# Attention by pair of heads and 192 tokens with stacked 64-query tiles; first layers in tiles of 192 and 384 tokens, second layers in 464; weights split in the first tile

## The reference

```python
def _attn_ref(q, k, v):                      # B, H, S, D = 4, 8, 576, 64; factor = 4
    q_d, k_d, v_d = (mean of each 4 tokens)  # 144 tokens
    out_up = np.repeat(sm_attn(q_d, k_d, v_d), factor, axis=2)
    mask = np.abs(pos[:, None] - pos[None, :]) < factor
    scores = np.where(mask, scale * np.matmul(q, k.transpose(0, 1, 3, 2)), -1e9)
    attn = softmax(scores)                   # divided by (sum + 1e-09)
    return out_up + np.matmul(attn, v)

def _moe_ref(x, w_in, w_out):                # 512 -> 2048 -> 512, ELU
    h = x @ w_in
    return np.where(h > 0, h, np.exp(np.minimum(h, 0)) - 1) @ w_out

def _moe2_ref(x, w_gate, w_val, w_out):      # 512 -> 1536 -> 512, SwiGLU
    g = x @ w_gate
    return (g / (1 + np.exp(-g)) * (x @ w_val)) @ w_out
```

## Time and profile before

| | |
|---|---|
| median of three runs | 1067.14 us |
| span of the profiled execution | 1064.6 us, clock 0.992 on average |
| the profiled execution's own time beside its span | not given apart; the median stands 2.5 us above the span |
| TensorE busy | 1020.6 us, 96% |
| DVE, ACT, POOL busy | 492.5, 383.6, 179.7 us |
| matmuls of first layers, 288 columns | 3072 |
| matmuls of second layers, 384 columns | 2592 |

### The profile page before, as it was taken

The page is one execution under the profiler, slowest core; times in us unless marked ns, Lnnn a source line. Parts: engine busy times, 40 slices in busy tenths (PEclk is TensorE's granted clock), DMA queues, the critical chain, the costliest instruction groups (busy, mean ns, idle before and its releaser), DMA issues.

```text
span 1064.6 us, 20019 instructions
## 1 busy us (share of the span) xinstructions
PE 1020.6 (96%) x7136; PEld 990.1 (93%) x7136; DVE 492.5 (46%) x1459; ACT 383.6 (36%) x1204; POOL 179.7 (17%) x207
## 2 busy tenths in 40 slices
PE   5499999899999999999999999999999999999998
PEld 4389999799998899999999999999999999999998
DVE  7856576365674555755644333223223232232222
ACT  5645344254453444545435622212212221221212
POOL 4740331001331012410007720000000000000000
PEclk9999999899999899999999999999999999999999
DMA  7621021111211111211034611000000001000000
GB/s 234 205 70 42 29 90 38 47 47 30 65 60 29 50 47 53 68 29 47 10 96 139 174 57 31 30 1 30 32 1 30 30 1 31 30 1 1 31 1 31
DMA packets 35146, 54.96 MB, mean 52 GB/s; under 512 B 3488, under 2 KB 23136, under 8 KB 35040
## 3 DMA queue, kind: packets, MB, share of 16 engines
q1 hardware_dynamic: 35040, 53.55, 16.7%
HBM read 44.10 MB, written 9.44 MB: 50 GB/s over the span
## 4 chain that ended last, share of the span: by engine, by line
PE 85%; DVE 6%; ACT 3%; issue 3%; DMA 1%; POOL 0%; SPq 0%; DVEq 0%; ACTq 0%
PE bank L314 26%; PE bank L315 25%; PE bank L316 25%; PE bank L274 3%; PE bank L300 2%; PE bank L285 1%; DVE g_sb L558 1%; PE bank L279 1%; PE bank L306 1%; ACT weights L704 1%; DVE prob L524 1%; DVE neg_max L509 1%; DVE v_pool L433 1%; DVE g_sb L560 1%; DVE prob L505 1%
## 5 line engine op out<-in xcount | busy, mean ns | idle before, releaser
L314 PE MATMUL bank<-x_hl,weights 128*128 128x384 f32 (+1 forms) x1088 | 352.1, 324 | 10.1 <-issue 9.6
L315 PE MATMUL bank<-x_hl,weights 128*128 128x384 f32 (+1 forms) x1088 | 347.5, 319 | 0.0
L316 PE MATMUL bank<-x_hl,weights 128*128 128x384 f32 (+1 forms) x1088 | 347.4, 319 | 0.0
L314 PEld LDWEIGHTS bank<-x_hl,weights 128*128 128x128 f32 x1088 | 206.2, 190 | 9.9 <-issue 8.7
L315 PEld LDWEIGHTS bank<-x_hl,weights 128*128 128x128 f32 x1088 | 206.5, 190 | 6.1 <-issue 6.1
L316 PEld LDWEIGHTS bank<-x_hl,weights 128*128 128x128 f32 x1088 | 206.3, 190 | 0.0
L314 PE MATMUL bank<-g_hl,weights 128*128 128x288 f32 x512 | 158.3, 309 | 1.5 <-DVE g_hl L566 1.5
L315 PE MATMUL bank<-g_hl,weights 128*128 128x288 f32 x512 | 152.7, 298 | 0.0
L316 PE MATMUL bank<-g_hl,weights 128*128 128x288 f32 x512 | 152.4, 298 | 0.0
L594 DVE TENSOR_TENSOR u_sb<-bank,u_sb 128x384 f32<-128x384 f32 x72 | 40.1, 557 | 199.3 <-ACT u_sb L744 199.3
L566 DVE TENSOR_TENSOR g_hl<-g_sb,g_hl 128x288 fp32r<-128x288 f32 x128 | 71.9, 562 | 86.6 <-ACT g_hl L681 86.6
(11 more groups left out here) (71 smaller groups left out, 1281.6 us busy)
## 6 DMA issues: line engine op xcount, KB each, us to landing
late_stages<-w SPq DMA_DIRECT2D x31, 256.0 KB, 3.2
v_win<-v_windows SPq DMA_DIRECT2D x32, 153.0 KB
q_sb<-qT SPq DMA_DIRECT2D x32, 144.0 KB, 2.2
k_sb<-kT SPq DMA_DIRECT2D x16, 288.0 KB, 3.0
v_raw<-v_rows SPq DMA_DIRECT2D x16, 288.0 KB
yT_scratch<-y_sb SPq DMA_DIRECT2D x32, 144.0 KB, 1.9
y_raw<-yT_scratch SPq DMA_DIRECT2D x6, 768.0 KB, 4.5
outT<-out_sb SPq DMA_DIRECT2D x24, 192.0 KB, 1.9
```

Source lines behind the costliest of these rows:

```text
L314: nc.tensor.matmul(bank[:, 0:n_cols], w_hi, x_hi, start=first, stop=False)
L315: nc.tensor.matmul(bank[:, 0:n_cols], w_hi, x_lo, start=False, stop=False)
L316: return nc.tensor.matmul(bank[:, 0:n_cols], w_lo, x_hi, start=False, stop=last)
```

## The change

Attention works on a unit: a pair of heads and 192 tokens, 48 units in all. The two heads of a pair are stacked on the 128 partitions, with 64 queries each, in three tiles with windows of 70 keys. One unit has 16 score instructions, 5 transposes of 128 columns and 20 output instructions. The mask is a tensor that DVE adds to the scores of all three tiles at once.

The prologue has only the first 4 units, the first 192 tokens. The first layers then run in seven tiles: 192, 192, and five of 384 tokens, with 16 steps each. All loops are written out. In the first tile, ACT and GpSimd also split two weight pieces in each step; only six are split before or at its start. The second layers run in four tiles of 464 tokens and one of 448.

In the slots, unit u has its scores at slot `at`, its normalisation on DVE at `at + 2`, its transposes at `at + 3` and its outputs at `at + 4`. Slots with even numbers stand between a hidden and an accumulate block, those with odd numbers behind the accumulate block. Units 4 to 7 are six slots apart, later ones four. The transposes of units 4 to 8 fall into the first tile, those of 9 to 16 into the second, those of 17 to 47 into wide tiles; the last tile has no attention.

```diff
-QT = 96
-NQ = 3
-T1 = SEQ // 2
-G_RING = 4
-STEPS = 2 * NF1
-T2 = 384
-NT2 = TOKENS // T2
+GROUP = 192
+GROUPS = TOKENS // GROUP
+THIRDS = SEQ // GROUP
+UNITS = GROUPS * PAIRS
+QT = 64
 WIN = QT + 6
+TILES = GROUP // QT
+LOC = TILES * WIN
+PQ = GROUP // POOL
+SCORES = LOC + SP
+LOCT = TILES * P
+POOLT = 2 * 2 * PQ
+TILE_GROUPS = [(0, 1), (1, 1), (2, 2), (4, 2), (6, 2), (8, 2), (10, 2)]
+NT1 = len(TILE_GROUPS)
+STEPS = NT1 * NF1
+WIDE1 = 2 * GROUP
+G_RING = 3
+T2 = 464
+STARTS2 = list(range(0, TOKENS, T2))
+WIDTHS2 = [min(T2, TOKENS - t) for t in STARTS2]
+NT2 = len(STARTS2)
-SLOT_OF_USE = [1, 1, 2, 4, 6, 8, 8, 10, 10, 11, 14, 15, 17, 17, 19, 19, 22, 22, 24, 25]
+PROLOGUE = PAIRS
+SLOT_S = {}
+for _u in range(PROLOGUE, UNITS):
+    if _u < 2 * PAIRS:
+        SLOT_S[_u] = 6 * (_u - PAIRS)
+    else:
+        SLOT_S[_u] = 2 * NF1 * (1 + (_u - 8) // 8) + 4 * ((_u - 8) % 8) - 6
+S_AT = {at: u for u, at in SLOT_S.items()}
+NORM_AT = {at + 2: u for u, at in SLOT_S.items()}
+T_AT = {at + 3: u for u, at in SLOT_S.items()}
+O_AT_SLOT = {at + 4: u for u, at in SLOT_S.items()}
...
-                for t in range(NQ):
-                    k0 = K0[NQ * h + t]
-                    nc.tensor.matmul(bank[0:QT, t * WIN:(t + 1) * WIN], q_sb[rows, pair % 2, t * QT:(t + 1) * QT],
-                                     k_sb[rows, pair % 2, k0:k0 + WIN], start=True, stop=True)
+            for t in range(TILES):
+                k0 = first_key(j * TILES + t)
+                for half in range(2):
+                    rows = slice(DH * half, DH * half + DH)
+                    nc.tensor.matmul(x[rows, t * WIN:(t + 1) * WIN], q_sb[rows, slot, t * QT:(t + 1) * QT],
+                                     k_sb[rows, slot, k0:k0 + WIN], start=True, stop=True)
...
+        def pe_transposes(pe, u):
+            x, y = bank_x(u), bank_y(u)
+            pe.wait_ge(ident_set, 1)
+            pe.wait_ge(normed, u + 1)
+            for t in range(TILES):
+                nc.tensor.transpose(x[0:WIN, t * P:(t + 1) * P], prob(u)[:, t * WIN:(t + 1) * WIN], ident[:, :])
+            if u >= PROLOGUE:
+                pe.wait_ge(x_done, u)
+            for kc in range(2):
+                mm = nc.tensor.transpose(y[0:SPH, kc * P:(kc + 1) * P],
+                                         prob(u)[:, LOC + kc * SPH:LOC + (kc + 1) * SPH], ident[:, :])
+            mm.then_inc(transposed_done, 1)
...
+        def pe_slot(pe, at):
+            if at in O_AT_SLOT:
+                pe_outputs(pe, O_AT_SLOT[at])
+            if at in S_AT:
+                pe_scores(pe, S_AT[at])
+            if at in T_AT:
+                pe_transposes(pe, T_AT[at])
...
-            with pe.Fori(0, BATCH - 1) as i:
-                pe_batch(pe, i, False)
-            pe_batch(pe, BATCH - 1, True)
-            with pe.Fori(0, NT2 // 2 - 1) as j:
-                pe_tiles2(pe, j, False)
-            pe_tiles2(pe, NT2 // 2 - 1, True)
+            pe_scores(pe, 0)
+            pe_scores(pe, 1)
+            pe_transposes(pe, 0)
+            pe_scores(pe, 2)
+            pe_outputs(pe, 0)
+            pe_transposes(pe, 1)
+            pe_scores(pe, 3)
+            pe_outputs(pe, 1)
+            pe_transposes(pe, 2)
+            pe_outputs(pe, 2)
+            pe_transposes(pe, 3)
+            pe_outputs(pe, 3)
+            pe_hidden(pe, 0)
+            pe_hidden(pe, 1)
+            for s in range(STEPS):
+                if s + 2 < STEPS:
+                    pe_hidden(pe, s + 2)
+                pe_slot(pe, 2 * s)
+                pe_accumulate(pe, s)
+                pe_slot(pe, 2 * s + 1)
+            pe_gate_val(pe, 0, 0)
...
+        def dve_masked_max(dve, u):
+            x, r = bank_x(u), u % 2
+            at = third_of(u)
+            dve.wait_ge(scores_done, u + 1)
+            if u >= PROLOGUE:
+                dve.wait_ge(transposed_done, u)
+            nc.vector.tensor_tensor(local_scores(u), x[:, 0:LOC].rearrange("q (t k) -> q t k", t=TILES),
+                                    mask[:, at:at + TILES, :], ALU.add).then_inc(masked, 1)
+            nc.vector.tensor_reduce(row_max[:, r, TILES:TILES + 1], x[:, LOC:SCORES], AXX, ALU.max)
+            dve.wait_ge(masked, u + 1)
+            nc.vector.tensor_reduce(row_max[:, r, 0:TILES], local_scores(u), AXX, ALU.max).then_inc(maxed, 1)
+            dve.wait_ge(maxed, u + 1)
+            nc.vector.tensor_tensor(neg_max[:, r, :], row_max[:, r, :], neg_scale[:, :], ALU.mult).then_inc(negmax_done, 1)
+        def dve_slot(dve, at):
+            if at in O_AT_SLOT:
+                dve_output(dve, O_AT_SLOT[at])
+            if at in S_AT:
+                dve_masked_max(dve, S_AT[at])
+            if at in NORM_AT:
+                dve_normalise(dve, NORM_AT[at])
...
+        def act_slot(act, at):
+            if at in S_AT:
+                act_exps(act, S_AT[at])
+            if at in O_AT_SLOT:
+                act_x_high(act, O_AT_SLOT[at])
+            if at in T_AT:
+                act_copies(act, T_AT[at])
...
+            act_exps(act, 0)
+            act_exps(act, 1)
+            act_copies(act, 0)
+            act_exps(act, 2)
+            act_weight_a(act, 0)
+            act_x_high(act, 0)
+            act_copies(act, 1)
+            act_exps(act, 3)
+            act_x_high(act, 1)
+            act_copies(act, 2)
+            act_weight_a(act, 1)
+            act_x_high(act, 2)
+            act_weight_a(act, 2)
+            act_copies(act, 3)
+            act_weight_a(act, 3)
+            act_x_high(act, 3)
+            for s in range(2):
+                act_weight_a(act, EARLY_A + s)
+                act_elu(act, s)
+                act_g_high(act, s)
+            for s in range(STEPS):
+                if s + 2 < STEPS:
+                    act_elu(act, s + 2)
+                act_slot(act, 2 * s)
+                if s + 2 < STEPS:
+                    act_g_high(act, s + 2)
+                act_slot(act, 2 * s + 1)
+                for i in range(EARLY_A + 2 + 2 * s, min(EARLY_A + 4 + 2 * s, N_PIECES_A)):
+                    act_weight_a(act, i)
+                if s % NF1 == NF1 - 1:
+                    act_y(act, s // NF1)
+                if s >= FIRST_B_STEP:
+                    act_weight_b(act, 2 * (s - FIRST_B_STEP))
+                    act_weight_b(act, 2 * (s - FIRST_B_STEP) + 1)
+                if s == FIRST_Y_SPLIT_STEP:
+                    act_split_y(act, 0)
+            act_swiglu(act, 0, 0)
...
+            for p in range(PAIRS):
+                pool_pool_v(pool, p)
+            pool_pool_qk(pool, PROLOGUE)
+            for i in range(EARLY_A + 2):
+                pool_weight_low(pool, i, ORDER_A[i], stage_a(i))
+            for s in range(STEPS):
+                pool_slot(pool, 2 * s)
+                pool_slot(pool, 2 * s + 1)
+                for i in range(EARLY_A + 2 + 2 * s, min(EARLY_A + 4 + 2 * s, N_PIECES_A)):
+                    pool_weight_low(pool, i, ORDER_A[i], stage_a(i))
```

More of the change, by code:

```diff
@@ new lines, in pe_slot, with three_passes @@
+        def pe_slot(pe, at):
[5 more added lines that the diff above has]
+                pe_transposes(pe, T_AT[at])
+        def three_passes(out, w_at, x_hi, x_lo, first, last):
+            w_hi, w_lo = w_at
+            nc.tensor.matmul(out, w_hi, x_hi, start=first, stop=False)
+            nc.tensor.matmul(out, w_hi, x_lo, start=False, stop=False)
+            return nc.tensor.matmul(out, w_lo, x_hi, start=False, stop=last)
@@ L593, in dve_swiglu @@
[L593 to L600 removed]
+            n, w = t * NF2 + f, WIDTHS2[t]
```

1095 lines of the change are left out of this document (497 added, 598 removed).

## The result

| | median us | runs | ratio to before |
|---|---|---|---|
| before | 1066.7 | 1065.4 to 1067.5 | |
| after | 1125.0 | 1110.4 to 1131.6 | 1.051 [1.047, 1.055] |

The change makes the kernel 58 us slower. The direction was forecast, and so was the wait of all 44 transposes; 1091 was 34 us short, and 1125 lies above the range (1039 to 1117). The profiled execution took 1124.8 us, span 1123.0. The run of 1131.6 us was a slow one, and the ratio leaves it out.

A forecast was written before the change was run, and what follows sets the result against it. TensorE was taken as the bound after the first 55 us, a DVE-TensorE chain before. Prologue 37, matmuls 414.5, attention 128, waits 50.5, clock 6, second layers 449.5 and tail 3.2 make 1088.7, plus 2.5 is 1091 us; range 1039 to 1117.

The forecast's parts named there:

- the wait of all 44 transposes: First layers: every transpose use waits for DVE's normalisation, about 0.6 us in wide tiles, 1 to 4 in the narrow ones.
- prologue: Before the first hidden block: four units' attention chain ends at 37 us (bounds 31 and 42), against 55.1 before.
- Four times 1, and 2 after the prologue: 6: First narrow tile and prologue's end: slow clock behind long TensorE waits loses 6 us in all.
- Rival 2: Narrow tiles: slow clock follows every wait, 12 times 2 us, instead of 6 in all; 1109 us, chance 0.13.
- GpSimd pooling stretches DVE for the 8 of them, +0.4 each: 3.2: Wide tiles: in eight units that start a batch, pooling lengthens DVE's work by 0.4 us each, 3.2 in all.
- First narrow tile 13.7: First 192-token tile: transposes wait 3.1 us four times and 1.3 for the fifth, with ACT late from weight casts.
- The second narrow tile: Second 192-token tile: ACT is late, eight transposes wait 1.35 us each, plus 1.4 once for y copies, 12.2 in all.
- the ordinary wide units: 384-token tiles: normalisation behind the ELU makes TensorE wait 0.6 us per unit, 18.6 us for 31 units.
- Attention 128: First layers: scores, transposes and outputs take TensorE 2.91 us per unit, 128 us for 44 units, against 118 before.
- Matmuls: First layers: 333.1 us at 384 columns plus 81.4 at 192 (pitch 0.106), 414.5 in all, 5.5 more than before.
- Second layers: Second layers: five tiles instead of six, with wider matmuls, take 449.5 us against 457.4, a gain of 7.9.
- The loops, 15 us: First layers: writing out the loops removes the backward jumps' issue waits and slow clock behind them, gaining about 15 us.

The follow-up runs named there:

- Filled waits: Changed kernel with extra 192-column matmuls, results unused, ahead of the transposes in the narrow tiles: 1101.9 us.
- v pooling late: Changed kernel with GpSimd's pooling of v moved behind the unit's normalisation: 1096.5 us.
- the last pair of experiments: three moves with normalisation in the scores' slot and weight-piece loads ahead of attention loads: 1043.6 us; with ACT's casts also ahead of the exponentials: 1036.5 us.
- three moves: Changed kernel, normalisation one slot earlier, first tile's transposes and outputs two slots later, v pooling started once the previous unit is normalised: 1047.9 us.
- the last kernel: three moves with normalisation in the scores' slot, weight-piece loads ahead of attention loads, and ACT's casts ahead of the exponentials: 1036.5 us.
- the experiment: Changed kernel with its second layers in six tiles of 384 tokens instead of 464: 1127.5 us.

## Why the prediction was wrong

Its sum, term by term, in spans (1088.7 forecast, 1123.0 measured):

| step | forecast | measured | |
|---|---|---|---|
| prologue | 37 | 33.4 | -3.6 |
| first-layer matmuls | 414.5 | 423.2 | +8.7 |
| attention on TensorE | 128 | 116.2 | -11.8 |
| transposes' waits (65.1), and other idle time | 50.5 | 67.3 | +16.8 |
| slow clock | 6 | 28.5 | +22.5 |
| second layers | 449.5 | 451.2 | +1.7 |
| tail | 3.2 | 3.2 | 0 |

- *"Four times 1, and 2 after the prologue: 6"* is the step that failed most: 28.5. I took 1 us for each of four waits. In the trace the clock stands at half for 10 to 14 us behind each of the four long waits (48.4 to 58.7, for instance), 3.5 to 4.5 us lost each. Four of the eight waits of the second tile have such a stretch too, 1.2 to 3.5 us lost, and three of the eight batch starts in wide tiles, 1.0 to 1.2. Rival 2 had the right mechanism and nearly the right size, 24 us for the clock, though not each of its 12 waits brings a stretch; it left out the attention work in these stretches, an estimated 10 us more (107.2 us from start to start, 96.8 for the same uses at full clock), which stands in the attention's row. Filled waits showed that the waits cause it.
- *"GpSimd pooling stretches DVE for the 8 of them, +0.4 each: 3.2"* was mis-sized by five: the eight waits sum to 20.3 us, 16.6 more than eight ordinary ones of 0.46. I treated the collision as a small stretch; it is a stop. In seven of the eight units it falls on the normalisation itself, on the first operation (1.39 to 1.59 us instead of 0.16, and the third 0.4 longer) or on the third (2.13 instead of 0.38, and the fourth 0.5 longer); in the eighth on the ELU operation ahead of it (2.21). v pooling late showed it.
- *First narrow tile 13.7*, measured 18.7 (4.05 to 4.47 a wait instead of 3.1). The order of ACT was right; that the cast waits for a load, queued behind attention loads on the sync engine, was in no term. Whether the piece load, the cast or GpSimd comes last changes from kernel to kernel, and only the last pair of experiments told them apart. The second narrow tile (12.2 against 14.2) and the ordinary wide units (0.6 against 0.46) were right.
- *Attention 128*: at full clock scores and outputs take 1.57 us together, transposes 0.62, and the first large matmuls behind them 0.19 more, 2.4 a unit and not 2.9. The outputs are what I had too dear. Scores alone take 0.85 us, and I had 0.88; outputs alone take 0.81, and I had kept the 1.21 of before because the 20 loads are the same, though their streams are now 64 and 48 columns instead of 96 and 72. Before has 118.5 by the same count. So the new attention seems to cost what the old did, but that is the waits' doing: with three moves it is 103.9 and in the last kernel 103.2, some 15 us cheaper than before.
- *Matmuls*: 192 columns have 0.1116 (0.106 forecast, inside its bounds), 384 in the first layers 0.1758 (0.1735 read from the second).
- *Second layers* came out nearly right in size, for a reason that the experiment contradicts: the gain is not the width of the tiles. In the kernel before the pitch there is 0.1743 in one tile and 0.1766 in the next, in turn, and 0.1733 in the changed kernel at the same 384 columns; the cause stays open.
- *The loops, 15 us*: right.

## What to carry to other kernels

Where a wait is forecast on TensorE, price three things: the missing time, the stretches at half clock behind it (16.8 us of loss went with 45 us of waits), and what any operation in the chain meets on GpSimd. A chain across three engines is set by the order on each: moving the normalisation, four operations of 1 us together, ahead of the ELU in DVE's order was worth 69 us here, more than the change gained everywhere else (22 in the prologue, 15 for the loops, 6 in the second layers). And when a stage is bound by a relay (load, cast, subtract), one link moved alone shows nothing or a loss; read who waits for whom in each queue, the sync engine's too, before moving it.

## What the hardware showed that was not expected

- A four-column DVE operation took 1.59 us instead of 0.16: it ended when the GpSimd addition beside it did. A product of 0.38 us took 2.13 in four batch-start units. Two operations of 0.38 and 0.29 us took 1.3 each.
- 276 more matmuls made the kernel 23 us faster, by keeping the clock at 2.4 GHz.
- Columns cost nearly the same at 384 and at 464: 0.451 and 0.454 ns each, though each matmul seemed to have a fixed part between 288 and 384.
